# Seven search visits of expert 0 re-placed, and its gathers and first weight piece asked sooner

## The chip, the cores and the metric
The kernel runs on one core of a Trainium2 chip. TensorE (PE) multiplies, VectorE (DVE), ScalarE (ACT) and GpSimd (POOL) work element by element, SyncE (SP) issues the large loads, and POOL issues the indirect ones (gathers and scatters by a list of row numbers). Each engine runs its own instructions in order; between engines, semaphores order the work. The metric is device time in microseconds. Before the change three runs took 818.77, 820.62 and 820.75 us, median 820.62. The profile is of one further execution, which took 818.85 us.

## The reference
Three layers follow each other:

```python
# 1. gated linear attention, 4 x 8 heads, 768 steps, head size 48
state = f[t] * state + outer(k[t], v[t]);  y[t] = q[t] @ state
# 2. mixture of experts: 3072 tokens, width 384, 8 experts, hidden 1024
order = argsort(-(x @ w_gate).flatten())
for idx in order:                       # greedy, each expert takes 384 tokens
    tok, e = idx // E, idx % E
    if assigned[tok] >= 0 or counts[e] >= cap: continue
    assigned[tok] = e; counts[e] += 1
out[mask_e] = relu(x[mask_e] @ w1[e]) @ w2[e]
# 3. one dense layer, hidden 2048
h = y @ w_in;  g = where(h > 0, h, exp(min(h, 0)) - 1);  out = g @ w_out
```

## The kernel before
Attention takes the first 134 us. Then the experts are worked through one by one, in the order in which they fill up; each takes 384 tokens through layers 2 and 3. Every float32 product is made of three products on rounded halves: hi x hi, low x hi and hi x low. ACT makes the `hi` parts (`t_hi`, `x_hi`, `y_hi`, `w1_hi` ...), and the `low` parts are differences that POOL (`t_lo`, and `w_out_low` and `w_in_low` once) and DVE (`w1_low`, `w2_low`, `x_lo`, `y_lo`) compute.

What PE does for one expert is written out by `order()` (line 997). `h m` is tile m of the hidden layer of expert k (9 products into a bank `m_ps`, lines 1390 to 1393), m from 0 to 7. `y m` adds hidden tile m to the expert's output (9 products, lines 1410 to 1412), one tile behind `h`, and waits for POOL's `t_lo` of that tile. The last two tiles, 6 and 7, are added in `y_end` 0, 1, 2 (lines 1425 to 1427), one for each third of the output, which ACT then rounds (`y_hi`, line 1207) and DVE lowers (`y_lo`, line 1543). `g01` and `g m` are the 16 tiles of the third layer's hidden values (lines 1450 to 1458), `o m` adds tile m to its output (lines 1470 to 1472), three tiles behind. The last three `o` of an expert run inside the next one's first `h`. `x` turns the next expert's gathered rows (line 1365).

Beside this runs the search for the next expert's tokens: six rounds that find a threshold digit by digit, then ties, places and the list of row numbers. It is a chain between PE and DVE. PE's side is cut into 16 visits (0 to 15), which `visits` places behind steps of the order. In round i visit 2i counts (`r_ps<-held,slot_hot`: 24 products for round 0, line 1304, six for the others, line 1300), DVE turns the counts into `reached`, visit 2i+1 adds these (one product, line 1309), and DVE reads the digit (line 1634), forms new limits (lines 1640, 1618) and compares (line 1569) for the next round. Visits 12 to 15 follow the digits; visit 15 gives the list, which DVE writes to `ids` (line 1742). A visit waits on PE for DVE's part, and DVE waits for each visit.

POOL, for each tile m of the third layer, first makes `whole` m (line 1119, when ACT has made `below` m), then `t_lo` m-1 (line 1091). In expert 0 it lowers `w_out` too (line 1102), two rows behind each `t_lo` of the hidden layer. From tile `gather_at` on it issues one of three gathers (line 1071) behind each tile, the first of them when `ids` is there. DVE, after the search for expert k+1 and the beginning of the search for k+2 (`begin`, `compare_halves`, line 100), waits for a number of `t_lo`s and then lowers expert k+1's weights and x. In expert 0 (`start`) the order is: piece 0 of `w1_low`, x part 0, pieces 1 and 2, x part 1, piece 0 of `w2_low`, x part 2, the other two pieces (lines 1554, 1548, 1560). In expert 0 the visits, this wait and `gather_at` have values of their own.

`visits_before_y` counts the visits that precede `y_end` 2 in the order; DVE lowers the three parts of y before it waits for the visit with that number.

Of the kernel before, what the change touches and what calls it, by code (L numbers as in the profile page):

```python
# [823 lines left out]
def route_and_feed(nc, block, sem, w1, w2, x_dram, w_in_raw, w_in_low, w_in_hi, w_in_upper, w_out_raw, w_out_low, logits, ident, w_out_loaded,  # L824
# [9 lines left out]
    KD, MH, MI, TT = width // P, hidden // P, w_in_low.shape[2] // P, cap // P  # L834
    NT = MH + MI
# [31 lines left out]
    with ExitStack() as ctx:  # L867
# [124 lines left out]
        lo_made = sem("lo_made")  # L992
# [10 lines left out]
        def order(start, routing, last):  # L1003

            steps = [("h", 0), ("h", 1), ("h", 2)]
            if not start:
                steps = [("o", MI - 3), ("h", 0), ("o", MI - 2), ("h", 1), ("o", MI - 1), ("h", 2)]
            steps += [("h", 3), ("y", 0)]
            for m in range(4, MH):
                steps += [("h", m), ("y", m - 3)]  # L1010
            steps += [("y", MH - 3)] + [("y_end", j) for j in range(KD)] + [("g01", 0)]
            for m in range(2, MI):
                steps.append(("g", m))
                back_of = [] if m < CATCH_UP - LAG - 1 else [m - LAG - 1] if m < CATCH_UP else [m - LAG - 1, m - LAG] if m == CATCH_UP else [m - LAG]
                steps += [("o", b) for b in back_of]
            if not routing:
                return steps
            if last:
                visits = {("h", 5): 0, ("h", 6): 1, ("y", 4): 2, ("g01", 0): 3}
            elif start:  # L1020
                visits = {("h", 3): 0, ("h", 4): 1, ("h", 5): 2, ("y", 2): 3, ("y", 3): 4, ("h", 7): 5, ("y", 5): 6, ("y_end", 0): 7,
                          ("g01", 0): 8, ("g", 2): 9, ("g", 4): 10, ("o", 0): 11, ("g", 6): 12, ("g", 7): 13, ("g", 8): 14, ("g", 9): 15}
            else:
                visits = {("h", 0): 0, ("o", MI - 2): 1, ("h", 2): 2, ("h", 3): 3, ("h", 4): 4, ("y", 1): 5, ("y", 2): 6, ("h", 6): 7,
                          ("h", 7): 8, ("y", 4): 9, ("y_end", 0): 10, ("y_end", 2): 11, ("g01", 0): 12, ("g", 3): 13, ("o", 0): 14, ("o", 2): 15}
            x_from = MI - LAG - KD if start else MI - LAG - KD - 1
            merged = []
            for step in steps:
                old = step[0] == "o" and step[1] >= MI - 3
                merged.append(step)  # L1030
                if step in visits:
                    merged.append(("visit", visits[step]))
                if step[0] == "o" and not old and x_from <= step[1] < x_from + KD:
                    merged.append(("x", step[1] - x_from))
            return merged

        def visits_before_y(start, last):
            steps = order(start, True, last)
            return sum(kind == "visit" for kind, _ in steps[:steps.index(("y_end", KD - 1))])
# [23 lines left out]
        def _(pool):  # L1063
            def gather(k, slot, t):
                if t == 0:
                    pool.wait_ge(list_ready, k + 1)

                    if not (isinstance(k, int) and k == 0):
                        pool.wait_ge(x_done, k * KD)
                    pool.sem_inc(pool_turn, 1)  # L1070
                nc.gpsimd.indirect_dma_start(out=x_rows[:, t, :], out_offset=None, in_=x_dram[:, :],
                                             in_offset=bass.IndirectOffsetOnAxis(ap=ids[slot][:, t:t + 1], axis=0),
                                             bounds_check=tokens - 1).then_inc(gathered[t], 16)

            def store(k, slot, apart=False):
                for t in range(TT):
                    if apart or t == 0:
                        pool.wait_ge(o_read, k * TT + (t + 1 if apart else TT))
                        pool.sem_inc(pool_turn, 1)
                    nc.gpsimd.indirect_dma_start(out=out[:, :], out_offset=bass.IndirectOffsetOnAxis(ap=ids[slot][:, t:t + 1], axis=0),  # L1080
                                                 in_=o_rows[t][:], in_offset=None,
                                                 bounds_check=tokens - 1).then_inc(stored, 16)

            def lower(k, n):

                if n < MH:
                    pool.wait_ge(h_read, k * MH + (n + 1))
                else:
                    pool.wait_ge(g_upper, k * MI + (n - MH + 1))
                pool.sem_inc(pool_turn, 1)  # L1090
                nc.gpsimd.tensor_tensor(t_lo[n % RING][:], whole[n % 3][:], t_hi[n % RING][:], ALU.subtract).then_inc(lo_made, 1)  # L1091
# [8 lines left out]
            def lower_w_out(row):  # L1100
                pool.wait_ge(w_out_upper, row // 4 + 1)
                nc.gpsimd.tensor_tensor(w_out_low[:, row, :], w_out_raw[:, row, :], w_out_hi[:, row, :], ALU.subtract).then_inc(fixed_lower, 1)

            def expert(k, slot, start, routing, last):
                gather_at = 9 if start else 3 if last else 7
                for n in range(MH):
                    lower(k, n)
                    if start:
                        for row in range(ROWS_AHEAD + 2 * n, min(ROWS_AHEAD + 2 * n + 2, MI - 1)):
                            lower_w_out(row)  # L1110
                    if not start and n == 3:
                        store(k + -1, 1 - slot)
                own = MI if routing else MI - HELPED
                for m in range(own + 1):
                    if m < own:
                        pool.wait_ge(below_ready, k * MI + (m + 1))
                        tile = whole[(MH + m) % 3]
                        pool.sem_inc(pool_turn, 1)
                        nc.gpsimd.tensor_tensor(tile[:], tile[:], below[m % 2][:], ALU.subtract).then_inc(g_made, 1)  # L1119
                    if m >= 1:  # L1120
                        lower(k, MH + m - 1)
                    if start and m == 1:
                        lower_w_out(MI - 1)
                    if routing and gather_at <= m < gather_at + TT:
                        gather(k + 1, 1 - slot, m - gather_at)
                        if m == gather_at + TT - 1:
                            pool.sem_inc(rows_asked, 1)
# [24 lines left out]
            for k in range(1, experts - 3, 2):  # L1152
                expert(k, 1, False, True, False)
                expert(k + 1, 0, False, True, False)
# [366 lines left out]
        def _(dve):  # L1521
# [28 lines left out]
            def lower_first(k, pieces=range(PIECES)):  # L1550
                for piece in pieces:
                    dve.wait_ge(w1_upper, k * PIECES + (piece + 1))
                    dve.sem_inc(dve_turn, 1)
                    v.tensor_tensor(w1_low[:, piece, :], w1_raw[:, piece, :], w1_hi[:, piece, :], ALU.subtract).then_inc(w1_split, 1)  # L1554
# [31 lines left out]
            def compare_halves():  # L1586
                for half in range(2):
                    compare_first(v, consts, scan, slice(half * tiles // 2, (half + 1) * tiles // 2), best_ps).then_inc(hit_ready, 1)
# [172 lines left out]
            def expert(k, slot, start, last):  # L1761

                search(k + 1, 1 - slot, visits_before_y(start, last), k, last)
                if not last:
                    begin(k + 2)
                    if not (isinstance(k, int) and k + 2 == experts - 1):
                        compare_halves()
                dve.wait_ge(lo_made, k * NT + MH + (12 if start else 6 if last else 10))
                if start:
                    lower_first(k + 1, [0])  # L1770
                    x_lower_part(k + 1, 0, r_ps)
                    lower_first(k + 1, range(1, PIECES))
                    x_lower_part(k + 1, 1, r_ps)
                    lower_second(k + 1, 0)
                    x_lower_part(k + 1, 2, r_ps)
                    lower_second(k + 1, 1)
                    lower_second(k + 1, 2)
                    return
                lower_first(k + 1)
                for m in range(KD):  # L1780
                    x_lower_part(k + 1, m, r_ps)
                    lower_second(k + 1, m)
# [75 lines left out]
```

## Time and profile before
| | us |
|---|---|
| three runs | 818.77, 820.62, 820.75 |
| the profiled execution | 818.85 |
| its span, first to last instruction | 816.9 |
| PE busy | 779.2 (95%) |
| POOL busy | 531.1 (65%) |
| ACT busy | 465.5 (57%) |
| DVE busy | 456.6 (56%) |

Times within the span count from its start. Attention ends at about 134 us, the search for expert 0's tokens at about 162, expert 0's own products run from 171 to about 253, those of the others from there to the end. The chain that ended last is by 85% PE. In a timeline row the first number is the start, the second the duration, and a bracket at the end tells how long the engine was idle before it and which instruction ended that. Consecutive products on PE overlap, so that their starts, not their durations, give the pace: 0.17 to 0.18 us for one of 128x384.

### The profile page before, as it was taken

To read this page: it belongs to the slowest core of one execution; us is meant where nothing else is said; L and a number is where in the kernel's file an instruction comes from. 1 tells how busy PE (TensorE), PEld (TensorE's weight loads), DVE (VectorE), ACT (ScalarE), POOL (GpSimd) and SP (SyncE) were. 2 spreads that over 40 slices of the span, in tenths; PEclk is the share of its full clock that TensorE was granted. 3 is DMA by queue.
4 is the path that set the end of the run, shared out by engine and by line. 5 is a ranking of instruction groups with operands and counts; after the bars stand their busy time and mean duration, and the time that the engine had idled before them with its cause. 6 is when DMAs were issued, how large, how long until landed. Compare 5 with 4: busy or idle time off the path is not lost.

```text
span 816.9 us, 17723 instructions
## 1 busy us (share of the span) xinstructions
PE 779.2 (95%) x5989; PEld 742.6 (91%) x5989; DVE 456.6 (56%) x1136; ACT 465.5 (57%) x980; POOL 531.1 (65%) x500
## 2 busy tenths in 40 slices
PE   7999996399999999999999999999999999999995
PEld 7888885389999999999999999999999999999995
DVE  6999997784665576358535863675365622330001
ACT  5777766052774287428733773377347635853653
POOL 8888882576875278528852885278538854954652
PEclk9999998599999999999999999999999999999998
DMA  6776692220130041004000400040004004100000
GB/s 197 215 219 209 197 337 99 102 92 2 63 123 1 30 155 30 11 21 164 21 23 7 166 19 30 4 173 10 30 22 153 11 30 154 30 1 31 1 1 29
DMA packets 33739, 65.68 MB, mean 80 GB/s; under 512 B 4560, under 2 KB 20944, under 8 KB 33280
## 3 DMA queue, kind: packets, MB, share of 16 engines
q1 hardware_dynamic: 27072, 50.36, 18.5%
q0 software_dynamic: 3136, 9.64, 3.6%
q10 hardware_dynamic: 3456, 4.72, 1.6%
q8 instruction: 43, 0.70, 0.4%
q14 instruction: 32, 0.26, 0.1%
HBM read 55.26 MB, written 9.44 MB: 79 GB/s over the span
## 4 chain that ended last, share of the span: by engine, by line
PE 85%; DVE 5%; POOL 3%; issue 3%; ACT 1%; SPq 1%; DMA 0%; DVEq 0%; ACTq 0%; POOLq 0%
PE o_ps L1470 8%; PE o_ps L1472 8%; PE o_ps L1471 8%; PE m_ps L1450 6%; PE m_ps L1454 6%; PE m_ps L1458 6%; PE o_ps L1410 3%; PE m_ps L1392 3%; PE o_ps L1412 3%; PE o_ps L1411 3%; PE m_ps L1390 3%; PE m_ps L1393 3%; PE a_ps L640 3%; PE y_ps L607 3%; PE xr_ps L583 2%
## 5 line engine op out<-in xcount | busy, mean ns | idle before, releaser
L1091 POOL TENSOR_TENSOR t_lo<-whole,t_hi 128x384 fp32r<-128x384 f32 x190 | 211.4, 1114 | 86.3 <-ACT t_hi L1176 84.4
L1119 POOL TENSOR_TENSOR whole<-whole,below 128x384 f32<-128x384 f32 x126 | 137.8, 1094 | 131.2 <-ACT below L1195 130.3
L1470 PE MATMUL o_ps<-w_out_hi,t_hi 128*128 128x384 f32 x378 | 127.7, 338 | 0.9 <-POOL t_lo L1091 0.8
L1472 PE MATMUL o_ps<-w_out_hi,t_lo 128*128 128x384 f32 x378 | 126.6, 335 | 0.0
L1471 PE MATMUL o_ps<-w_out_low,t_hi 128*128 128x384 f32 x378 | 126.4, 334 | 0.0
L1450 PE MATMUL m_ps<-y_hi,w_in_hi 128*128 128x384 f32 x288 | 99.6, 346 | 0.0
L1454 PE MATMUL m_ps<-y_hi,w_in_low 128*128 128x384 f32 x288 | 96.6, 335 | 0.0
L1191 ACT ACTIVATE whole<-m_ps 128x384 f32<-128x384 f32 x96 | 47.0, 490 | 64.9 <-PE m_ps L1458 62.3
L1175 ACT ACTIVATE whole<-m_ps 128x384 f32<-128x384 f32 x48 | 23.6, 492 | 94.5 <-PE m_ps L1390 81.0
L1195 ACT ACTIVATE below<-below 128x384 f32<-128x384 f32 x128 | 67.3, 526 | 16.8 <-ACT below L1192 0.8
L1470 PEld LDWEIGHTS o_ps<-w_out_hi,t_hi 128*128 128x128 f32 x378 | 71.0, 188 | 2.2 <-issue 1.7
L1554 DVE TENSOR_TENSOR w_low<-w_raw,w_hi 128x1024 fp32r<-128x1024 f32 x24 | 39.8, 1708 | 56.0 <-POOL t_lo L1091 55.7
L1471 PEld LDWEIGHTS o_ps<-w_out_low,t_hi 128*128 128x128 f32 x378 | 71.0, 188 | 0.0
L1472 PEld LDWEIGHTS o_ps<-w_out_hi,t_lo 128*128 128x128 f32 x378 | 71.0, 188 | 0.0
L1183 ACT CAST t_hi<-whole 128x384 fp32r<-128x384 f32 x128 | 63.9, 499 | 10.4 <-POOL whole L1119 9.3
L1458 PE MATMUL m_ps<-y_lo,w_in_hi 128*128 128x384 f32 x288 | 64.2, 334 | 0.0
L1450 PEld LDWEIGHTS m_ps<-y_hi,w_in_hi 128*128 128x128 f32 x288 | 54.2, 188 | 0.0
L1454 PEld LDWEIGHTS m_ps<-y_hi,w_in_low 128*128 128x128 f32 x288 | 54.2, 188 | 0.0
L1410 PE MATMUL o_ps<-t_hi,w_hi 128*128 128x384 f32 x144 | 51.4, 357 | 1.2 <-POOL t_lo L1091 1.2
L1458 PEld LDWEIGHTS m_ps<-y_lo,w_in_hi 128*128 128x128 f32 x288 | 51.3, 188 | 0.0
L1392 PE MATMUL m_ps<-x_hi,w_hi 128*128 128x384 f32 x144 | 49.9, 346 | 0.0
L1412 PE MATMUL o_ps<-t_lo,w_hi 128*128 128x384 f32 x144 | 48.5, 337 | 0.0
(278 smaller groups left out, 1882.7 us busy)
## 6 DMA issues: line engine op xcount, KB each, us to landing
w_raw<-w SPq DMA_DIRECT2D x16, 1536.0 KB, 6.4
f_in<-f_t SPq DMA_DIRECT2D x48, 96.0 KB, 2.3
k_in<-k_t SPq DMA_DIRECT2D x48, 96.0 KB, 2.4
q_in<-q_t SPq DMA_DIRECT2D x48, 96.0 KB, 2.4
v_in<-v_rows SPq DMA_DIRECT2D x24, 192.0 KB, 2.7
x_scratch<-x_row ACTq DMA_DIRECT2D x24, 192.0 KB, 2.6
w_in_raw<-w_in SPq DMA_DIRECT2D x1, 3072.0 KB, 11.5
w_out_raw<-w_out SPq DMA_DIRECT2D x1, 3072.0 KB, 21.0
```

The lines of the kernel that those rows point to most:

```text
L1091: nc.gpsimd.tensor_tensor(t_lo[n % RING][:], whole[n % 3][:], t_hi[n % RING][:], ALU.subtract).then_inc(lo_made, 1)
L1119: nc.gpsimd.tensor_tensor(tile[:], tile[:], below[m % 2][:], ALU.subtract).then_inc(g_made, 1)
L1195: nc.scalar.activation(below[m % 2][:], below[m % 2][:], ACT.Relu, bias=1.0, scale=-1.0).then_inc(below_ready, 1)
L1392: nc.tensor.matmul(m_ps[m % RING][:], w1_hi[:, t, cols], x_hi[:, t, :], start=(t == 0), stop=False)
L1410: nc.tensor.matmul(o_ps[j][:], w2_hi[:, m, cols], hi[:], start=(m == 0), stop=False)
L1412: ins = nc.tensor.matmul(o_ps[j][:], w2_hi[:, m, cols], lo[:], start=False, stop=False)
L1450: ins = nc.tensor.matmul(bank[:], w_in_hi[:, t, cols], y_hi[:, t, :], start=(t == 0), stop=False)
L1454: nc.tensor.matmul(bank[:], w_in_low[:, t, cols], y_hi[:, t, :], start=False, stop=False)
L1458: ins = nc.tensor.matmul(bank[:], w_in_hi[:, t, cols], y_lo[:, t, :], start=False, stop=(t == KD - 1))
L1470: nc.tensor.matmul(o_ps[t][:], hi[:, rows], w_out_hi[:, m, :], start=(m == 0), stop=False)
L1471: nc.tensor.matmul(o_ps[t][:], hi[:, rows], w_out_low[:, m, :], start=False, stop=False)
L1472: ins = nc.tensor.matmul(o_ps[t][:], lo[:, rows], w_out_hi[:, m, :], start=False, stop=(m == MI - 1))
```

## The change
Three edits, all for expert 0 alone. Visits 1 to 7 of the search for expert 1 get other places in PE's order. POOL asks for expert 1's rows behind tiles 8, 9, 10 in place of 9, 10, 11. DVE's wait before it lowers expert 1's weights is for the tenth `t_lo` of the third layer in place of the twelfth.

```diff
@@ order(): the visits of expert 0
-  visits = {("h", 3): 0, ("h", 4): 1, ("h", 5): 2, ("y", 2): 3, ("y", 3): 4, ("h", 7): 5, ("y", 5): 6, ("y_end", 0): 7,
+  visits = {("h", 3): 0, ("y", 1): 1, ("y", 2): 2, ("h", 6): 3, ("h", 7): 4, ("y", 4): 5, ("y_end", 0): 6, ("y_end", 2): 7,
             ("g01", 0): 8, ("g", 2): 9, ...
@@ expert() on POOL
-                gather_at = 9 if start else 3 if last else 7
+                gather_at = 8 if start else 3 if last else 7
@@ expert() on DVE
-                dve.wait_ge(lo_made, k * NT + MH + (12 if start else 6 if last else 10))
+                dve.wait_ge(lo_made, k * NT + MH + (6 if last else 10))
```

PE, the end of expert 0's hidden layer, before (`o_ps0` and `o_ps1` are the first two thirds of the output, `t_hi2` and `t_hi3` the tiles 6 and 7; the rows are 331 to 340 of its order):

```order
331 L1300 MATMUL r_ps<-held,slot_hot 128x32 x6
332 L1425 MATMUL o_ps0<-t_hi2,w2_hi 128x384
333 L1426 MATMUL o_ps0<-t_hi2,w2_low_2434 128x384
334 L1427 MATMUL o_ps0<-t_lo2,w2_hi 128x384
335 L1425 MATMUL o_ps0<-t_hi3,w2_hi 128x384
336 L1426 MATMUL o_ps0<-t_hi3,w2_low_2434 128x384
337 L1427 MATMUL o_ps0<-t_lo3,w2_hi 128x384
338 L1309 MATMUL r_ps<-reached_5,ones 128x8
339 L1425 MATMUL o_ps1<-t_hi2,w2_hi 128x384
```

The same place in the changed kernel:

```order
331 L1425 MATMUL o_ps0<-t_hi2,w2_hi 128x384
332 L1426 MATMUL o_ps0<-t_hi2,w2_low_2434 128x384
333 L1427 MATMUL o_ps0<-t_lo2,w2_hi 128x384
334 L1425 MATMUL o_ps0<-t_hi3,w2_hi 128x384
335 L1426 MATMUL o_ps0<-t_hi3,w2_low_2434 128x384
336 L1427 MATMUL o_ps0<-t_lo3,w2_hi 128x384
337 L1300 MATMUL r_ps<-held,slot_hot 128x32 x6
338 L1425 MATMUL o_ps1<-t_hi2,w2_hi 128x384
```

Visit 6, the six products, stood ahead of `y_end` 0 and now stands behind it; visit 7, the one product, has left this place for the end of `y_end` 2.

DVE at the same time, difference of its order:

```order
 L1628 TENSOR_TENSOR room_left<-room_left,r_ps 32x8 x2
 L1630 TENSOR_TENSOR reached_5<-r_ps,room_left 31x8
-L1634 TENSOR_REDUCE digit<-r_ps 128x1
-L1640 TENSOR_SCALAR prefix<-digit,prefix 128x1
-L1618 TENSOR_SCALAR r_ps<-ways,prefix,order_mask 128x32
-L1569 TENSOR_TENSOR slot_hot<-best,r_ps 128x768
 L1543 TENSOR_TENSOR y_lo<-o_ps0,y_hi 128x384
 L1543 TENSOR_TENSOR y_lo<-o_ps1,y_hi 128x384
 L1543 TENSOR_TENSOR y_lo<-o_ps2,y_hi 128x384
+L1634 TENSOR_REDUCE digit<-r_ps 128x1
+L1640 TENSOR_SCALAR prefix<-digit,prefix 128x1
+L1618 TENSOR_SCALAR r_ps<-ways,prefix,order_mask 128x32
```

The digit of visit 7 and the comparison that follows from it are now computed behind the three `y_lo`.

POOL in tiles 8 to 11 of the third layer, before (the ring of `t_lo` and of `whole` is numbered by buffer, so `t_lo0` is tile 8 here):

```order
132 L1119 TENSOR_TENSOR whole2<-whole2,below1 128x384
133 L1091 TENSOR_TENSOR t_lo0<-whole1,t_hi0 128x384
134 L1071 DMA x_rows<-x_scratch,ids1 128x384
135 L1119 TENSOR_TENSOR whole0<-whole0,below0 128x384
136 L1091 TENSOR_TENSOR t_lo1<-whole2,t_hi1 128x384
137 L1071 DMA x_rows<-x_scratch,ids1 128x384
```

and with the change:

```order
132 L1071 DMA x_rows<-x_scratch,ids1 128x384
133 L1119 TENSOR_TENSOR whole2<-whole2,below1 128x384
134 L1091 TENSOR_TENSOR t_lo0<-whole1,t_hi0 128x384
135 L1071 DMA x_rows<-x_scratch,ids1 128x384
136 L1119 TENSOR_TENSOR whole0<-whole0,below0 128x384
137 L1091 TENSOR_TENSOR t_lo1<-whole2,t_hi1 128x384
138 L1071 DMA x_rows<-x_scratch,ids1 128x384
```

The first gather now stands ahead of `whole` 9 and `t_lo` 8, and each of the three one tile sooner.

## Rows read from the trace of the kernel before

**Rows 1.** Page, part 2: granted PE clock in tenths, 40 equal slices.

```profile
PEclk9999998599999999999999999999999999999998
```

**Rows 2.** Waits of PE, 162 to 290 us (us in total, times, longest).

```profile
PE o_ps L1410 <- POOL t_lo L1091: 1.2, 1, 1.2
PE o_ps L1470 <- POOL t_lo L1091: 0.6, 1, 0.6
```

**Rows 3.** Chain of waits near 197 us (start, us, what).

```profile
195.69 1.95 POOL t_lo L1091 x2
...
197.78 0.41 PE o_ps L1425
```

**Rows 4.** Timeline of PE, 196 to 204 us (start, us, engine, line, operation, out<-in).

```profile
196.68 0.32 PE L1300 MATMUL r_ps<-held,slot_hot 128*128 128x32 bf16 x6
...
197.29 0.34 PE L1427 MATMUL o_ps<-t_lo,w_hi 128*128 128x384 f32 x1
...
198.38 0.18 PE L1309 MATMUL r_ps<-reached,ones 128*128 128x8 bf16 x1
...
198.68 0.34 PE L1426 MATMUL o_ps<-t_hi,w_low 128*128 128x384 f32 x1
...
200.44 0.33 PE L1427 MATMUL o_ps<-t_lo,w_hi 128*128 128x384 f32 x1
...
203.74 0.32 PE L1300 MATMUL r_ps<-held,slot_hot 128*128 128x32 bf16 x6
```

**Rows 5.** Timeline of DVE and ACT, same stretch.

```profile
198.61 0.17 DVE L1634 TENSOR_REDUCE digit<-r_ps 128x1 int32<-128x8 f32 x1 [0.84 <-PE r_ps L1309]
...
199.48 0.95 DVE L1569 TENSOR_TENSOR slot_hot<-best,r_ps 128x768 bf16<-128x768 f32 x1
...
200.89 0.48 ACT L1207 CAST y_hi<-o_ps 128x384 fp32r<-128x384 f32 x1 [0.56 <-PE o_ps L1427]
```

**Rows 6.** Timeline of ACT and DVE at the same place in expert 1.

```profile
282.66 0.48 ACT L1207 CAST y_hi<-o_ps 128x384 fp32r<-128x384 f32 x1 [0.57 <-PE o_ps L1427]
...
283.28 0.56 DVE L1543 TENSOR_TENSOR y_lo<-o_ps,y_hi 128x384 fp32r<-128x384 f32 x1 [0.49 <-ACT y_hi L1207]
...
283.76 0.16 DVE L1634 TENSOR_REDUCE digit<-r_ps 128x1 int32<-128x8 f32 x1
```

**Rows 7.** Timeline of POOL, 229 to 248 us.

```profile
229.15 1.03 POOL L1119 TENSOR_TENSOR whole<-whole,below 128x384 f32<-128x384 f32 x1 [3.00 <-ACT below L1195]
...
231.29 1.02 POOL L1071 DMA_INDIRECT x_rows<-x_scratch,ids  x1
...
232.70 1.02 POOL L1119 TENSOR_TENSOR whole<-whole,below 128x384 f32<-128x384 f32 x1 [0.39 <-issue]
...
234.84 1.03 POOL L1071 DMA_INDIRECT x_rows<-x_scratch,ids  x1
...
235.89 1.04 POOL L1119 TENSOR_TENSOR whole<-whole,below 128x384 f32<-128x384 f32 x1
...
247.41 2.11 POOL L1091 TENSOR_TENSOR t_lo<-whole,t_hi 128x384 fp32r<-128x384 f32 x1
```

**Rows 8.** Timeline of ACT and PE, 238 to 241 us.

```profile
238.66 0.50 ACT L1183 CAST t_hi<-whole 128x384 fp32r<-128x384 f32 x1
...
240.03 0.33 PE L1470 MATMUL o_ps<-w_out_hi,t_hi 128*128 128x384 f32 x1
```

**Rows 9.** Timeline of DVE, 228 to 242 us.

```profile
228.38 0.17 DVE L1742 CAST ids<-ids_f 128x3 int32<-128x3 f32 x1
...
233.66 3.42 DVE L100 TENSOR_TENSOR slot_hot<-r_ps,limit 128x1536 bf16<-128x1536 f32 x2
...
241.28 1.23 DVE L1554 TENSOR_TENSOR w_low<-w_raw,w_hi 128x1024 fp32r<-128x1024 f32 x1 [4.20 <-POOL t_lo L1091]
```

**Rows 10.** Timeline of DVE and PE at visit 14.

```profile
221.84 0.21 DVE L1668 TENSOR_TENSOR_SCAN listed<-r_ps,zero_t 128x24 bf16<-128x24 f32 x1
...
222.20 0.16 PE L1319 MATMUL r_ps<-listed,before 128*128 128x1 bf16 x1
```

## The prediction

> **What bounds the kernel now.** I read the page's two upper parts first: PE is busy 779.2 of 816.9 us and at nearly full clock outside the first search and the end [rows 1], so a gain has to be time in which PE waits inside the experts. The view of waits for PE between 162 and 290 us [rows 2] leaves little of that in the stretch that the change touches: 1.2 us before the products of output tile 1 of expert 0, and 0.6 us before the first leftover product of expert 0's output layer, at 249.67 us. Both end with POOL's `t_lo`. The chain of waits gives a third, too short to be listed there: in `y_end` 0, the products of tile 7 begin 0.14 us after POOL's last `t_lo` of the hidden layer [rows 3]. Without it they would have begun one step (0.17 us) after 197.29 [rows 4], at 197.46; they begin at 197.78. So from 178 to 197.6 us POOL, which lowers `w_out` between its `t_lo`, releases PE twice, and after that PE runs gapless up to 249 us.
>
> **The search visits.** A visit is PE work inside PE's order, and it may not make PE wait: what DVE computes between two visits must be done when PE arrives. I take its cost on PE from the rows. Visit 6 (six products) starts at 196.68, and the third product behind it starts at 197.29: 0.61, less two steps of 0.175, is 0.26 us. Visit 7 (one product) starts at 198.38 and the second product behind it at 198.68: 0.30 less 0.17 is 0.13 us [rows 4]. No visit is added or removed; what counts is on which side of PE's two waits a visit lies.
>
> Visit 1 stood inside the 1.2 us wait for tile 1 (h4, visit, y1) and now follows y1. It filled idle time and cost nothing; y1 still starts when POOL lets it, so the visit's 0.13 us now falls behind. Visit 6 stood before `y_end` 0 and now stands behind it. So on PE between the two waits 0.13 comes in and 0.26 goes, PE reaches tile 7 of `y_end` 0 at 197.46 - 0.26 + 0.13 = 197.33, and still goes on at 197.78, because POOL's string of operations ends when it did. POOL is not moved by any of this: its `t_lo` need h5 to h7, which shift by at most 0.13 us, and POOL comes to them later than they are ready. Behind the second wait PE now has visit 6 as well: **+0.26 us** at the start of `g01`. Visit 7 (now behind `y_end` 2) was behind the wait already and costs nothing by its move. If POOL's string came out shorter, the term would fall towards 0.13, not below.
>
> Do the moved visits wait for DVE? From the result of a digit visit to the end of its comparison DVE needs 0.23 (198.38 to 198.61), 0.87 (to 199.48) and 0.95, together 2.05 us [rows 4, 5]. Visit 2 now comes 18 products (3.1 us) after visit 1, visit 4 comes 18 after visit 3, visit 6 comes 15 (2.6 us) after visit 5. The first round has three short steps more (some 0.6 us), which leaves it 0.5. Visits 3 and 5 stand nine products behind 2 and 4, the distance that visits 2 and 3 had before, without a wait. Covered, all of them.
>
> Visit 8, which itself stays behind `g01`, is the tight one. DVE now lowers the three parts of y before it takes visit 7's digit, where before it had done that comparison first. The last product of `y_end` 2 started at 200.44; it now starts at 200.44 + 0.26 - 0.13 = 200.57. ACT's last `y_hi` began 0.45 behind it (200.89) [rows 4, 5]. In expert 1, where the same order stands already, the last `y_lo` begins 0.62 after that `y_hi` and the digit 0.48 later [rows 6]. Then 0.87 and 0.95 as above, and 0.14 for the release: 200.57 + 0.45 + 0.62 + 0.48 + 0.87 + 0.95 + 0.14 = 204.08. PE arrives at 203.74 + 0.26 = 204.00. **+0.08 us**; bounds 0 (the estimate is that close) and 0.3, if a step meets a POOL operation. Everything behind is moved by the 0.34 us as a whole, PE, ACT, DVE and the load of expert 1's weights alike.
>
> **The gathers.** All times here are those of before, without the common 0.34. DVE has the list at 228.38 + 0.17 [rows 9], so a gather asked at tile 8 starts no sooner than 228.70, 2.6 us before the old one at 231.29. POOL, in order, has been idle since 226.15 (3.00 before 229.15) and would stand in that wait, and behind it stands `whole` of tile 9, which was ready for its old start of 229.15. A first gather takes 1.41 with what follows (231.29 to 232.70), a later one 1.05 (234.84 to 235.89), and `whole`, `t_lo` and the way to the next gather take 2.14 (229.15 to 231.29) [rows 7]. So: gather 228.70, `whole` 9 230.11 (0.96 late), gather 232.25, `whole` 10 233.30 (0.60 late), gather 235.44, `whole` 11 236.49 (0.60 late), `t_lo` 10 at 237.47; then the three gathers are over and POOL is level again. Who waits? ACT wants `whole` 11 at 238.66, and PE wants `t_lo` 10 at 240.03 [rows 8]; the second has about 1.5 us of cover, tiles 8 and 9 more. The rows come sooner, but x is turned only behind product o10, where PE did not wait for them. Worth **0**.
>
> **The weights.** DVE's wait for the 12th `t_lo` becomes one for the 10th. Only piece 0 of `w1_low` can use that: x part 0 stands next in DVE's order and needs ACT's `x_hi`, which comes from a turn on PE that has not moved. And DVE is not free before 233.66 + 3.42 = 237.08 [rows 9]. The piece (1.23 us at 241.28) therefore moves to about 237.1 and lands beside POOL's `whole` 11 and `t_lo` 10 instead of beside `whole` 13. A POOL operation that takes 1.04 us (235.89) took 2.11 (247.41) where DVE lowered weights [rows 7], 1.1 us more. With `whole` 11 from 236.49 to 237.5 and the piece behind it, `t_lo` 10 ends at about 239.7 and PE is released at 239.85, before 240.03: **0**, with 0.2 us of cover left. The 0.6 us wait at 249.67 stays: it is made by pieces 1 and 2, which stand behind x part 0 as before.
>
> That last reckoning has a rule behind it. The Trainium skill, page "SBUF — State Buffer", section "Who interferes with whom", says that a DVE instruction with two SBUF inputs contends with a GpSimd instruction that reads SBUF, and that whoever starts first holds the port for its whole instruction. The 2.11 us row agrees. By it the order of arrival decides: `whole` 11 first gives no cost, the piece first gives the rival below. The same page's section on the sides of SBUF warns that DVE can starve POOL's descriptors; here a gather beside DVE's comparison took its usual 1.03 us [rows 7, 9], so it changes no term.
>
> **Sum.** 0.26 + 0.08 = 0.34 us slower. The profiled execution took 818.85 us (span 816.9 and 1.95 around it), so 819.2. The three runs shown were 818.77, 820.62 and 820.75; their median is 1.8 above the profiled one, and against it the forecast is 820.62 + 0.34 = 821.0 us. I call 0.3% (2.5 us) what a measurement of this kernel can tell from no change.
>
> **Rivals.**
> 1. *The piece of w1 gets the port first (slower).* It is asked at 237.1; if `whole` 11 starts later than that (each gather with 1.41 instead of 1.05 would put it at 237.2), `whole` 11 ends at about 239.3. ACT's `t_hi` of tile 11 is late by 0.7, and since ACT has no idle time from there to `x_hi` part 0, that is late too, then pieces 1 and 2, then the `t_lo` at 247.41. PE's wait at 249.67 grows by 0.7, at most by one more hold of 1.1: total 1.0 to 1.5 us, **822.0**. For: only 0.6 us lie between the two starts. Against: later gathers follow at 1.05. It decides from `whole` 11 at 237.1 on.
> 2. *The phase of the search (slower).* Visit 14 was released by DVE's `listed`, which ended at 222.05, 0.15 before the visit began [rows 10]; no slack. If the 0.08 us at visit 8 makes one DVE step just miss the port and wait out a POOL operation (1 us), PE waits as long: **822.0** (820.62 + 0.34 + 1.0).
> 3. *POOL's relief (faster).* `whole` 13 is no longer stretched, and DVE's port is free around 241. If that carries through to the `t_lo` at 247.41, the 0.6 us wait goes: 820.62 + 0.34 - 0.6 = **820.4**. Against: `whole` 14 waits for ACT's `below`, which waits for PE. If the wait for tile 1 went as well, 1.2 more: 819.2.
> 4. *The change does nothing at all*: wait 2 absorbs more than I think, **820.6**.
>
> **How the numbers follow.** Forecast 0.62, rival 1 0.13, rival 2 0.08, rival 3 0.07, rival 4 0.10. No case alone reaches 2.5 us. The runs themselves spread over 2 us, so a median of three may fall at either end: 818.9 + 0.3 at the low, 820.75 + 1.5 at the high. Range 818.5 to 822.4. Slower by over 0.3% needs rivals 1 and 2 together with a high draw: 0.05. Faster by over 0.3% needs rival 3 in full and a low draw: 0.04. Within: 0.91.
>
> **What would show it.** On PE of the changed kernel: the wait before y1 a little over 1.2, no wait at visits 1 to 7, tile 7 of `y_end` 0 at 197.8, `g01` at 200.9, visit 8 at about 204.1 with at most 0.1 of waiting. On POOL: some 2.5 us of idle time ended by `ids` before the first gather, and the `t_lo` of tile 10 done before PE reaches o10. On DVE: piece 0 at about 237.5, pieces 1 and 2 where they were. Wrong would be: visit 8 held for half a microsecond or more, ACT's `x_hi` part 0 late against PE's turn, or a wait at 249.67 other than 0.6. A difference outside expert 0 would be one that I don't foresee.

## The result

The changed kernel took 820.65 us (median of 22 runs), the kernel before 818.67 us (22 runs beside them). The ratio is 1.0024, 95% interval 1.0018 to 1.0030: slower by 2.0 us, clear of the noise and inside the 0.3% that I had called no change. The time forecast was 821.0, but that it came out near is luck, since two errors cancel: the median of the three runs shown before the change, 820.62, was 1.95 us above what many runs give, and my 0.34 us for the change was 1.6 us too low. Against the profiled execution of before (818.85) that of the changed kernel took 820.57, with a span of 818.6.

The waits of PE in the changed kernel, from 162 us to the end (us in total, times, longest):

```profile
PE m_ps L1458 <- issue: 1.5, 1, 1.5
PE o_ps L1410 <- POOL t_lo L1091: 1.1, 1, 1.1
PE o_ps L1470 <- POOL t_lo L1091: 0.6, 2, 0.4
...
```

The first line is new, beside those of [rows 2]. The releaser "issue" says that PE waited for nothing that the profile shows, in the middle of the products of tile 10 of the third layer. The timeline of PE there:

```profile
230.00 0.33 PE L1450 MATMUL m_ps<-y_hi,w_in_hi 128*128 128x384 f32 x1
230.17 0.33 PE L1454 MATMUL m_ps<-y_hi,w_in_low 128*128 128x384 f32 x1
232.04 0.68 PE L1458 MATMUL m_ps<-y_lo,w_in_hi 128*128 128x384 f32 x3 [1.53 <-issue]
```

By the pace of the products the last line should start at 230.35; it starts 1.69 us later, and the spans differ by 1.7. The kernel has no semaphore wait between these instructions. What does stand near is a packet of the queue that the page names q8, instruction: 43 packets with 0.70 MB in a span, 16 KB each. The page does not say whose instructions they are; that this one is PE's is read from the waits that follow it. Two cuts of the DMA view, each 0.1 to 0.2 us wide, hold one such packet (columns: packets, MB, share of 16 engines). Before, 226.7 to 226.8 us:

```profile
q8 instruction: 1, 0.02, 69.2%
```

and with the change, 229.5 to 229.7 us:

```profile
q8 instruction: 1, 0.02, 34.7%
```

It starts at 226.71 before and at 229.59 now and takes 1.1 us in both; in the changed kernel PE goes on 1.3 us after its end. The load of expert 1's w1 and w2 (one issue each, 1.5 MB each) keeps the DMA engines at work from 220.7 to about 230. So the reading is that PE ran out of instructions, because their next block came at the end of that load instead of in its midst.

What I had forecast is in the trace as well. This execution runs 0.21 us ahead of the one before from 171 us on (y1 starts at 183.00, before at 183.21). The timeline of PE around `y_end` 0 and visit 8, answering to [rows 4]:

```profile
197.56 0.41 PE L1425 MATMUL o_ps<-t_hi,w_hi 128*128 128x384 f32 x1 [0.21 <-POOL t_lo L1091]
...
198.16 0.32 PE L1300 MATMUL r_ps<-held,slot_hot 128*128 128x32 bf16 x6
...
200.53 0.18 PE L1309 MATMUL r_ps<-reached,ones 128*128 128x8 bf16 x1
...
203.88 0.38 PE L1300 MATMUL r_ps<-held,slot_hot 128*128 128x32 bf16 x6
```

and that of DVE:

```profile
201.44 0.56 DVE L1543 TENSOR_TENSOR y_lo<-o_ps,y_hi 128x384 fp32r<-128x384 f32 x1 [0.49 <-ACT y_hi L1207]
...
202.78 0.95 DVE L1569 TENSOR_TENSOR slot_hot<-best,r_ps 128x768 bf16<-128x768 f32 x1
```

Visit 8 at 203.88 is where 204.08 less 0.21 puts it, 0.15 us behind the comparison that ends at 203.73. POOL at the gathers, answering to [rows 7]:

```profile
229.66 1.02 POOL L1071 DMA_INDIRECT x_rows<-x_scratch,ids  x1 [3.25 <-ACT t_hi L1183]
230.71 1.01 POOL L1119 TENSOR_TENSOR whole<-whole,below 128x384 f32<-128x384 f32 x1
```

and DVE, answering to [rows 9]:

```profile
228.57 0.17 DVE L1742 CAST ids<-ids_f 128x3 int32<-128x3 f32 x1
...
236.81 1.22 DVE L1554 TENSOR_TENSOR w_low<-w_raw,w_hi 128x1024 fp32r<-128x1024 f32 x1
```

The first gather starts 0.9 us after the list is there (228.74), not 0.15, and `whole` 9 follows it at 230.71. The releaser that its row names is not the one that counts: in e7_sp_later below, ACT's `t_hi` ended only as the gather started, and the gather was again 0.93 us behind the list. Nobody waited for these.

### The profile page after: what moved, and what is told of

Its sections match the earlier page's. It is cut to its first block, busy times and chain, and to the rows that moved or that the text cites. A ratio compares the mean times of both kernels' runs of the same rounds, so it can differ in the third digit from the quotient of the medians.

```text
span 818.6 us, 17723 instructions
## 1 busy us (share of the span) xinstructions
PE 779.5 (95%) x5989; PEld 742.5 (91%) x5989; DVE 456.7 (56%) x1136; ACT 465.4 (57%) x980; POOL 530.6 (65%) x500
## 4 chain that ended last, share of the span: by engine, by line
PE 85%; DVE 6%; POOL 3%; issue 3%; ACT 1%; SPq 1%; DMA 0%; DVEq 0%; ACTq 0%; POOLq 0%
PE o_ps L1470 8%; PE o_ps L1472 8%; PE o_ps L1471 8%; PE m_ps L1450 6%; PE m_ps L1454 6%; PE m_ps L1458 6%; PE o_ps L1410 3%; PE m_ps L1392 3%; PE o_ps L1412 3%; PE m_ps L1390 3%; PE o_ps L1411 3%; PE m_ps L1393 3%; PE a_ps L640 3%; PE y_ps L607 2%; PE last_bank L1450 2%
## 5 line engine op out<-in xcount | busy, mean ns | idle before, releaser
L1458 PE MATMUL m_ps<-y_lo,w_in_hi 128*128 128x384 f32 x288 | 64.2, 334 | 1.5 <-issue 1.5
L1458 PEld LDWEIGHTS m_ps<-y_lo,w_in_hi 128*128 128x128 f32 x288 | 51.3, 188 | 1.7 <-issue 1.7
```

What stands on the lines that cost most here:

```text
L1458: ins = nc.tensor.matmul(bank[:], w_in_hi[:, t, cols], y_lo[:, t, :], start=False, stop=(t == KD - 1))
```

## The experiments

**Theory F**: the 2 us are a block of PE's instructions that comes late behind the load of expert 1's weights, and the change causes it only by shifting PE a few tenths against that load. **Rival G**: the sooner gathers hold the block up. **Rival H**: the moved visits cost it by themselves.

### The three edits apart

`e1_visits` is the line of `visits` alone, `e2_gather` is `gather_at = 8`, `e3_lower` is DVE's wait alone, each on the kernel before, as in the diff of the change.

e1_visits: 

> The kernel before with the seven visits alone. Theory F: the 2.0 us come from one block of PE's instructions that arrives late (1.5 us wait of PE before L1458 at 232.04, released by nothing that the profile shows; the 16 KB instruction packet of that queue starts at 229.59 in place of 226.71), and the moved visits bring that about by shifting PE by a few tenths against the load of expert 1's weights. Then this run is slower than before by 1.5 to 2.1 us with the same wait. Rival G: the sooner gathers hold up the block; then this run shows only my 0.1 to 0.35 us of the visits and no such wait.

e2_gather: 

> The kernel before with the gathers one tile sooner alone. Theory F: no change (within 0.2 us) and the instruction packet near 226.7, since the first gather is issued only at about 229 us. Rival G: slower by 1.5 to 2 us, with the 1.5 us wait of PE.

e3_lower: 

> The kernel before with the sooner lowering of the first weight piece alone. Both F and G: within 0.2 us of before; piece 0 at about 237.1, no change of PE's wait at 249.67.

Against 818.67 for before: visits 820.84 us (ratio 1.0026, interval 1.0015 to 1.0038), gathers 818.49 (0.9998, 0.9989 to 1.0007), lowering 818.49 (the same ratio and interval). The visits carry it all. In their trace the wait is there again:

```profile
PE m_ps L1458 <- issue: 1.5, 1, 1.5
```

with the packet at 230.48 in an execution that runs 0.8 us behind that of the changed kernel (y1 at 183.83). In the gathers' trace the packet starts at 226.51 and there is no such wait. G has fallen.

One expectation missed without moving the time. In e3_lower PE's wait at 249.67 was to stay; it is gone. In its place PE waits 0.48 us, up to 242.22, for the rows of the last gather, which took 1.83 us beside piece 0 (at 236.98, 1.97 us) where it took 1.03 before.

### Less load ahead of the block

```diff
+                if isinstance(k, int) and k == 1:
+                    sp.wait_ge(mm_done, MH + 10)
+                    sp.sem_inc(load_turn, 1)
                 sp.dma_start(w2_raw[:], ...)
```

> The changed kernel, with the load of expert 1's w2 held until the products of tile 9 of the third layer are done (about 227 us), so that less load traffic stands ahead of the instruction block. Theory F: the packet starts before 228, the 1.5 us wait goes, and the time is 0.0 to 0.4 us above before (818.7 to 819.1); w2 lands near 232, before it is wanted at 236. Rival G: the wait stays and the time stays 2 us above before.

Measured 818.81 us, ratio 1.0000 (0.9991 to 1.0009); the packet starts at 227.97, and no wait at L1458. All three edits of the change are in, so the visits by themselves do not cost 2 us: H has fallen too. What is left above before is 0.14 us.

The trace holds something that a block waiting behind the load's packets does not explain. The last packets of w1 start just before 226, and w2 is issued only at 227.84. The DMA view from 226 to 227.9 us:

```profile
DMA packets 0, 0.00 MB, mean 0 GB/s; under 512 B 0, under 2 KB 0, under 8 KB 0
```

and from 227.9 to 228.1 us:

```profile
q8 instruction: 1, 0.02, 29.2%
```

No packet of any queue starts for 1.9 us, and only then comes the block. It was not waiting for its turn among the load's packets in that stretch; what it was waiting for, no view shows.

### Shifting PE's stream and the load against each other

```diff
 # e5_pe_pad (on the changed kernel), e10_before_pad (on the kernel before)
             for n in range(VISITS_FIRST):
+                if n >= 12:
+                    for _ in range(4):
+                        pe.sem_inc(pe_turn, 1)
                 visit(0, n)
 # e6_warm27 (on the kernel before)
-                keep_warm(30)
+                keep_warm(27)
 # e7_sp_later (on the changed kernel), e12_before_sp (on the kernel before)
+                if isinstance(k, int) and k == 1:
+                    for _ in range(6):
+                        sp.sem_inc(load_turn, 1)
                 sp.dma_start(w1_raw[:], ...)
```

e5_pe_pad: 

> The changed kernel with 16 more semaphore increments in PE's stream, in the idle time of the first search. They move no work, but every later instruction stands 16 places further on, so that PE comes to the point where its next block is asked for earlier by some 1.2 us, clear of the issue of expert 1's weights at 219.84. Theory F (a race between the block's request and the load): the 1.5 us wait goes, 818.7 to 819.2. Rival H (the moved visits cost the 1.5 us by themselves, the packet's place being a coincidence): stays at 820.6.

e6_warm27: 

> The kernel before with 27 in place of 30 products that only keep PE busy while it waits for the first gathers: six instructions fewer in PE's stream ahead of the experts, no visit moved, so the same point of the stream is reached some 0.4 us later against the load. Theory F: the instruction packet near 229.5 and the 1.5 us wait of PE without any part of the change: 820.3 to 820.8. Rival H: 818.7 as before.

e7_sp_later: 

> The changed kernel with six semaphore increments on SP ahead of the issue of expert 1's w1 load, so that both loads are issued 0.2 to 0.4 us later and nothing else moves. In the traces the w1 issue stands 0.04 to 0.07 us earlier against PE's products in the runs with the wait than in those without. Theory F in its sharp form (that order decides): no wait, 818.7 to 819.2. If the race is with something else than the issue of the loads: 820.6.

These ran on a chip on which the kernel before itself falls into two groups: 23 runs around 818.55 and 12 from 820.2 to 822.4. On the other two chips 1 of 29 and none of 27 runs of before were in the upper group.

- e5_pe_pad: 818.90 us, all 12 runs from 818.4 to 819.4. No run of the changed kernel stands beside these; against its 820.65 above, sixteen idle instructions, far from the place, took 1.75 us off. The packet starts at 226.69. The waits of PE, 162 to 290 us:

```profile
PE o_ps L1410 <- POOL t_lo L1091: 1.0, 1, 1.0
PE o_ps L1470 <- POOL t_lo L1091: 0.5, 1, 0.5
PE o_ps L1425 <- POOL t_lo L1091: 0.2, 1, 0.2
```

- e6_warm27: 820.22 us; 11 of 12 runs from 819.7 to 820.6, one at 818.9, which is the profiled one (packet at 226.29). So no trace shows the late block in this kernel, nor in a run of before from the upper group; that it stands behind them is inferred from the 2 us. No part of the change is in it. 11 of 12 against 12 of 35 for before on the same chip; the ratio of medians, 1.0008 (0.9998 to 1.0018), says less, since both are mixtures.
- e7_sp_later: 822.55 us, ratio 1.0031 (1.0020 to 1.0042), all 12 runs above 820.8. The load was issued 0.4 us later, the packet started at 230.08, and the wait grew (the edit moves the line numbers by 3):

```profile
PE m_ps L1461 <- issue: 2.1, 1, 2.1
```

The wait grew by 0.6 us only; the rest is PE's clock. The granted clock fell behind that wait, in the view of windows from 233.6 to 237.0 us (third number from the end):

```profile
233.60:237.00 3.40, 3.40 (x13) 3.40 (x12) 3.33 (x2) 2.60 (x5) 2.12 (x3) 0.50 0.23 63
```

0.50 is the lower of the clock's two levels, 1.2 of 2.4 GHz. PE's products follow each other there at 0.32 us in place of 0.17, which costs some 1.6 us. With the 0.6 this makes the 2.1 us by which the profiled span, 820.7, lies above the changed kernel's 818.6. Behind the waits of 1.5 us, in the changed kernel and in e1_visits, the granted clock stayed at 1.00.

The sharp form of F, in which the order of the request and the issue decides, has fallen: a later load did not help.

e10_before_pad: 

> The kernel before with the 16 increments of e5_pe_pad in PE's stream. The runs of before fall into two groups, near 818.5 and near 820.6. Theory F: with the request 1.2 us earlier all runs are in the lower group, 818.3 to 819.0. If the increments have nothing to do with the groups, about a third of the runs stay near 820.6.

e12_before_sp: 

> The kernel before with the six increments on SP ahead of the issue of w1, which put the load 0.4 us later against PE's products. With the changed kernel that lengthened the wait from 1.5 to 2.1 us. If a later load makes the block later in general, this run falls into the upper group, 820.6 to 821.2; if the sharp form of F held (a later load helps), all runs are near 818.5.

e10_before_pad: 818.58 us, ratio 1.0001 (0.9992 to 1.0010). e12_before_sp: 818.67 us, ratio 1.0004 (0.9995 to 1.0013), one of 11 runs at 821.3. Both tell little of the groups, because on this chip before had no upper group. e12 does say that the 0.4 us alone does not bring the late block about on this chip.

### Where the block stands without a load

```diff
+                if isinstance(k, int) and k == 1:
+                    sp.wait_ge(mm_done, MH + 9)
+                    sp.sem_inc(load_turn, 1)
                 sp.dma_start(w1_raw[:], ...)
```

> The kernel before with both loads of expert 1's weights held until the products of tile 8 of the third layer are done (about 222.2 us), some 2.5 us later. It shows where PE's instruction packet stands when no load is under way. Theory F: it starts between 219 and 224 us, ahead of the load's first packets (about 224.3), and no PE wait at L1458. A rival would be that the packet is asked for only at 226 us or later whatever the load does: then it stays at 226.7. The time itself may rise by 1 to 2 us, since ACT stands waiting for w1 until about 229.

The DMA view from 223.5 to 223.7 us:

```profile
q8 instruction: 1, 0.02, 34.2%
```

The packet starts at 223.57, just ahead of the first of the load's (223.63), 3.1 us sooner than in before and 6.0 sooner than in the changed kernel. PE's stream is the same as in before up to there (visit 14 at 222.20 in both). So the block is asked for by then, and a load that is already under way holds it back, by 3 or by 6 us; by what means, e4_w2_later leaves open. The time was 821.67 us (4 runs, ratio 1.0050, 1.0034 to 1.0065), from other waits, of which the longest new one is

```profile
PE r_ps L1368 <- DMA x_rows<-x_scratch,ids: 1.5, 1, 1.5
```

and another, for `x_hi`, takes 0.6 us.

### A version that beats both

The two waits of PE for POOL in the hidden layer of expert 0 are there because POOL lowers `w_out` between its `t_lo`. `e8_pool` moves these rows to where POOL idles, on the kernel before; `e11_pool_pad` adds the 16 increments.

```diff
-   for row in range(ROWS_AHEAD + 2 * n, min(ROWS_AHEAD + 2 * n + 2, MI - 1)):
+   behind = {1: (4, 6), 2: (6, 8), 3: (8, 10), 4: (10, 12), 7: (12, 15)}
+   for row in range(*behind.get(n, (0, 0))):
        lower_w_out(row)
```

e8_pool: 

> The kernel before with POOL's lowering of w_out re-placed: no rows behind the first t_lo, two each behind the second to fifth, three behind the eighth, where POOL then waits 7.6 us. It should take away both waits of PE for POOL in the hidden layer of expert 0 (1.15 and 0.31 us): 817.1 to 817.4, by every theory, if the instruction block is in time; 2 us more if the shift loses that race.

e11_pool_pad: 

> POOL's re-placed w_out rows and the 16 increments together, on the kernel before: 816.8 to 817.4 in every run, without the upper group (818.9 to 819.4) that e8_pool showed in 4 of 12.

e8_pool: 817.20 us, ratio 0.9976 (0.9964 to 0.9988), 8 runs from 816.7 to 817.6 and 4 from 818.9 to 819.4, the two groups again. e11_pool_pad: 816.98 us, ratio 0.9980 (0.9971 to 0.9989), 11 runs from 816.5 to 817.5. That is 1.54 us under before beside it and 3.7 under the changed kernel's 820.65; the two waits were 1.15 and 0.3. Of the waits from 162 to 290 us one is left, 0.7 us for POOL at 248.09, the old one of 249.67.

Whether the increments keep the upper group away was not tested where it is frequent: e11 ran on a chip on which before had none.

## Why the prediction was right or wrong

**The visits' 0.26 us: right.** PE waited at tile 7 of `y_end` 0 for POOL as before, visit 6 stands behind it, and `g01` follows 0.17 later than before once the 0.21 is taken off; the rest of the 0.26 falls behind visit 7.

**Visit 8's 0.08 us: right.** It started 0.01 us from the place forecast. Together, PE is 0.35 us later at visit 8 than in before, once the 0.21 is taken off. With the late block out of the way, the whole change costs 818.90 against 818.55 (e5_pe_pad against the lower group of before beside it), 0.35 us, and 818.81 against 818.67 in e4_w2_later.

**The gathers, 0: right in effect, wrong by 0.8 us in a term.** I let a gather that waits start 0.15 us after the list; it took 0.9. The cover was enough. The run with the gathers alone shows no loss.

**The weights, 0: right.** The piece moved from 241.28 to 236.81 and met POOL's gather, since POOL had been pushed back by the late block and DVE had not. The wait at 249.67 went from 0.63 to 0.42 us (251.37 now). Rivals 1 and 2 did not occur; 3 occurred for 0.2 us at most. This trace did not test rival 1, but that of e5_pe_pad, without the late block, does. DVE and POOL there:

```profile
237.22 3.42 DVE L1557 TENSOR_TENSOR w_low<-w_raw,w_hi 128x1024 fp32r<-128x1024 f32 x1
...
237.57 1.02 POOL L1119 TENSOR_TENSOR whole<-whole,below 128x384 f32<-128x384 f32 x1
```

The piece is ahead of `whole` 11 by 0.35 us, which is the rival's condition, and its price does not follow: `whole` 11 and `t_lo` 10 kept their 1.02 us, the piece was stretched from 1.23 to 3.42, and only `whole` 12 took 1.99. PE's wait was 0.46 us, not more than the 0.63 before.

**The step that failed** is the sentence behind visit 8: "Everything behind is moved by the 0.34 us as a whole". It holds for what the semaphores order. PE's instructions come by DMA too, and that was in the page before the change (43 packets on q8, 0.70 MB) and in none of my terms. 1.69 us of PE's delay, of the 2.0 measured, are this block. In the three traces with the wait PE goes on 2.4 to 2.5 us after the start of the packet, so the wait follows the packet. It is shown that a load under way sets the block back, that the visits alone bring the late block about, and that 16 instructions ahead or a later w2 remove it. It is not shown what decides between early and late. There are two places and nothing between: 6.1 to 7.2 us behind the issue of w1 in the nine traces without the wait in which the two loads follow each other as in before, 9.8 us in the three with it. Later load: the packet still late with the change, no effect without it; fewer instructions: late, by the times alone; more: early. A simple race between one request and one issue does not give all of these, and the records hold no time of the request.

The Trainium skill, page "Runtime: NRT & Kernel Launch", section "Instruction fetch mechanics", says that an engine's instructions are refilled in blocks of 256 over a DMA queue of its own while it works on the block before, and that the cost is mostly hidden. The packets of 16 KB agree; hidden it was in before and not in the changed kernel.

**The base.** I took the median of three, 820.62, as the kernel's level. Two of those three were in the upper group, as were 3 of 22 in all. The profiled execution, 818.85, was the better guide, and its distance to the median was a sign: something in this kernel has two outcomes 2 us apart. The stated range, 818.5 to 822.4, is also not what its own terms give: 818.9 + 0.3 is 819.2, and 820.75 + 1.5 is 822.25.

## What to carry to other kernels

Where run times fall into two groups, find what differs before you price an edit of a few tenths: an edit can be right to 0.01 us in its own terms and flip the kernel into the other group. Look for waits with no releaser, and lay the packets of the instruction queues beside the large loads. To tell such a cause from the edit's own cost, shift the instruction stream by a handful of idle instructions and time it again. And look at the granted clock behind a long wait before you put the whole loss down to the wait.

## What I had not expected of the hardware

- An instruction block of PE that needs 1.1 us started at 223.57 with no load under way. With a 3 MB load under way it started 3 us later (226.71) or 6 us later (229.59), in the other traces likewise 6.1 to 7.2 or 9.8 us behind the issue of the load.
- With the second half of the load held back, the block started at 227.97, behind 1.9 us in which no DMA packet started at all.
- After a wait of 2.1 us PE's granted clock was 0.50 from about 233.7 to 236.9 us; after waits of 1.5 us, in two other traces, it stayed at 1.00.
- PE went on 1.3 us after the end of the block's packet (230.70 to 232.04 in the changed kernel).
- A gather on POOL that waits for its list starts 0.9 us after the list is written (228.74 to 229.66, and 0.92 to 0.93 in four other traces), against 0.15 us behind POOL's own work [rows 7].
- The share of runs in the upper group of the same kernel was 12 of 35, 1 of 29 and 0 of 27 on three chips.
